# The two single tiles of a fused attention and two-MLP kernel become narrower and join the pairs of the second MLP

## What is computed

```python
qn = q / (norm(q, axis=1) + 1e-6); kn = k / (norm(k, axis=1) + 1e-6)
a = softmax(kn.T @ qn / tau); x = (v @ a)           # [6016, 256]
g = x @ w_gate; x = (silu(g) * (x @ w_val)) @ w_out  # first MLP, 1536 wide
h = x @ w_in2;  out = (h * clip(h + 3, 0, 6) / 6) @ w_out2  # second MLP, 2048 wide
```

## Time and profile before

| | |
|---|---|
| profiled execution | 1092.75 us |
| its span (first to last instruction) | 1090.8 us |
| median of the three timed runs | 1092.9 us |
| PE busy | 1083.8 us (99%), 4890 matmuls |
| DVE, ACT, POOL busy | 787.8, 637.9, 318.3 us |
| DMA | 46.81 MB, of 115417 packets 96528 under 512 B |
| granted TensorE clock | 1.00 |

### The profile page before, as it was taken

The page is one execution under the profiler, slowest core; times in us unless marked ns, Lnnn a source line. Parts: engine busy times, 40 slices in busy tenths (PEclk is TensorE's granted clock), DMA queues, the critical chain, the costliest instruction groups (busy, mean ns, idle before and its releaser), DMA issues.

```text
span 1090.8 us, 14296 instructions
## 1 busy us (share of the span) xinstructions
PE 1083.8 (99%) x4890; PEld 905.2 (83%) x4890; DVE 787.8 (72%) x1160; ACT 637.9 (58%) x1113; POOL 318.3 (29%) x232
## 2 busy tenths in 40 slices
PE   9999999999999999999999999999999999999999
PEld 7888988888888888888877878888888888888888
DVE  6788777667666766756688786776776776776776
ACT  8731245665665566566566776676676676665322
POOL 7999462200210220223087432122121121000000
DMA  9711112002002100101122200020020020020210
GB/s 380 247 34 20 39 34 40 1 1 65 13 1 58 20 1 21 38 1 42 56 59 65 90 1 19 21 39 21 20 39 23 17 39 20 1 40 14 39 20 16
DMA packets 115417, 46.81 MB, mean 43 GB/s; under 512 B 96528, under 2 KB 105104, under 8 KB 115344
## 3 DMA queue, kind: packets, MB, share of 16 engines
q1 hardware_dynamic: 114768, 44.71, 15.2%
q10 hardware_dynamic: 576, 1.18, 0.3%
HBM read 33.55 MB, written 12.32 MB: 42 GB/s over the span
## 4 chain that ended last, share of the span: by engine, by line
PE 95%; DVE 2%; issue 1%; DMA 0%; ACT 0%; ACTq 0%; DVEq 0%
PE psum L1639 42%; PE psum L1650 34%; PE psum L1542 5%; PE psum L1563 4%; PE psum L1552 4%; PE psum L1420 2%; PE psum L1524 2%; PE psum L1596 1%; DVE prod L1146 1%; PE psum L1452 1%; PE psum L1433 0%; PE psum L1594 0%; PE psum L1577 0%; DMA qk_first<-in_k 0%; DVE slots L1274 0%
## 5 line engine op out<-in xcount | busy, mean ns | idle before, releaser
L1650 PE MATMUL psum<-prod,down_w 128*128 128x512 f32 x1680 | 412.9, 389 | 0.0
L1650 PEld LDWEIGHTS psum<-prod,down_w 128*128 128x128 f32 x1680 | 315.4, 188 | 65.5 <-DVE y_right L1298 0.2
L1639 PE MATMUL psum<-x_even,up_w 128*128 128x512 f32 x1092 | 267.0, 390 | 2.7 <-DVE slots L1278 2.6
L1639 PE MATMUL psum<-x_odd,up_w 128*128 128x512 f32 x1008 | 245.5, 390 | 0.5 <-DVE more_slots L1320 0.5
L1639 PEld LDWEIGHTS psum<-x_even,up_w 128*128 128x128 f32 x1092 | 204.2, 188 | 47.3 <-DVE slots L1278 5.0
L1639 PEld LDWEIGHTS psum<-x_odd,up_w 128*128 128x128 f32 x1008 | 189.0, 188 | 40.6 <-DVE more_slots L1320 1.2
L1278 DVE TENSOR_TENSOR slots<-psum,slots 128x512 f32<-128x512 f32 x100 | 68.7, 687 | 55.4 <-ACT slots L921 33.3
L1269 DVE TENSOR_TENSOR slots<-psum,slots 128x512 f32<-128x512 f32 x80 | 55.2, 690 | 73.9 <-PE psum L1639 73.6
L1146 DVE TENSOR_TENSOR prod<-slots,prod 128x512 fp32r<-128x512 f32 x120 | 90.9, 766 | 21.1 <-ACT prod L889 21.1
L1324 DVE SCALAR_TENSOR_TENSOR prod<-slots,prod 128x512 fp32r<-128x512 f32 x120 | 85.8, 715 | 26.5 <-ACT prod L967 22.5
L1320 DVE SCALAR_TENSOR_TENSOR slots<-slots 128x512 f32<-128x512 f32 x100 | 72.2, 722 | 32.0 <-ACT slots L977 32.0
(11 more groups left out here) (177 smaller groups left out, 1403.5 us busy)
## 6 DMA issues: line engine op xcount, KB each, us to landing
out<-out_sb SPq DMA_DIRECT2D x45, 128.0 KB, 2.7
v_in<-in_v SPq DMA_DIRECT2D x44, 128.0 KB, 3.3
qk<-in_q SPq DMA_DIRECT2D x8, 512.0 KB, 9.2
qk<-in_k SPq DMA_DIRECT2D x7, 512.0 KB, 10.7
x_odd_raw<-y_rows SPq DMA_DIRECT2D x12, 256.0 KB, 3.2
y_rows<-act_out SPq DMA_DIRECT2D x10, 256.0 KB, 2.1
y_rows<-y_right SPq DMA_DIRECT2D x10, 256.0 KB, 3.0
x_even_raw<-y_rows SPq DMA_DIRECT2D x10, 256.0 KB, 3.2
```

What stands on the lines that cost most here:

```text
L1639: end = mm(bank, w[:, u, k, part, :], XS[pair % 2][:, k, m, :], start=start and (part, m) == PASSES[0], stop=stop and (part, m) == PASSES[-1],
L1650: end = mm(SUMS_OUT[2 * side + h], w[:, j, part, h * P:(h + 1) * P], buffer_of(f, x)[:, m, :], start=start and (part, m) == PASSES[0], sto ...
```

## The change

The tiles at the two ends of the order become two equal ones: ALONE = (6016 - 10 x 512) / 2 = 448 tokens, at tokens 0 and 448. The ten tiles of the pairs follow them. In the first MLP both still run singly, with 448 where there were 512 and 384. In the second MLP the two form a sixth pair of 448-token tiles, which runs second (pair NARROWER = PAIRS + 1); `second_alone`, `up2`, `down_rows`, `finish_rows` and the weights kept for them (`row2_w`) go away. Every helper of a frame cuts its buffers to `pair_width`. The last pair (LAST_PAIR, 512 tokens wide) now ends the kernel: `finish_second` runs the downs of its last frame, `turn_last` transposes all four sums from PSUM, and `store` writes them, the left tile by SP, the right tile by SP (two DMAs) and ACT (two).

```diff
-    TILES = N // BANK
-    LAST = N - TILES * BANK
+    PAIRS = N // (2 * BANK)
+    ALONE = (N - 2 * PAIRS * BANK) // 2
...
-    FRAMES = SECOND + PAIRS * FRAMES2
+    FRAMES = SECOND + (PAIRS + 1) * FRAMES2
+    NARROWER, LAST_PAIR = PAIRS + 1, 2 * PAIRS
...
+    def pair_width(pair):
+        return ALONE if pair == NARROWER else BANK
...
+        def store(queue, pair, side, groups=range(GROUPS)):
+            queue.wait_ge(out_ready, 2 * KC * (pair - PAIRS) + KC * (side + 1))
+            for g in groups:
+                queue.dma_start(tile(out, tile_of(pair, side))[g],
+                                out_sb[g * SQUARE:(g + 1) * SQUARE, side, 0:pair_width(pair) // SQUARE * KC, :]).then_inc(out_stored, 16)
...
-            load_y_alone(1)
-            store(TILES - 2, 0, 4 * PAIRS - 2)
-            store(TILES - 1, 1, 4 * PAIRS)
-            store(0, 0, 4 * PAIRS + KC)
-            store_block(sp, 1)
+            for pair in range(PAIRS, LAST_PAIR):
+                if pair + 2 <= LAST_PAIR:
+                    load_y(pair + 2 - PAIRS)
+                store(sp, pair, 0)
+                store(sp, pair, 1)
+            store(sp, LAST_PAIR, 0)
+            store(sp, LAST_PAIR, 1, range(2))
...
-            second_alone(0)
-            second_alone(1)
-            act.wait_ge(out_stored, 16 * GROUPS * TILES)
-            for b in range(LAST_BLOCKS):
-                act.wait_ge(low_summed, b + 1)
-                nc.scalar.copy(out_rows(b), ROWS[b][:, C:2 * C]).then_inc(low_kept, 1)
-            for b in (0, 2):
-                store_block(act, b)
+            store(act, LAST_PAIR, 1, range(2, GROUPS))
...
+            def turn_last(side):
+                for h in range(KC):
+                    dve.wait_ge(z_summed, KC * side + h + 1)
+                    nc.vector.transpose(out_sb[:, side, h::KC, :],
+                                        sums_out(LAST_PAIR, side, h).rearrange("p (m t) -> p m t", t=SQUARE)).then_inc(out_ready, 1)
...
-                    mm(bank, w[:, u, k, part, :], XS[pair % 2][:, k, m, :],
+                    mm(bank, w[:, u, k, part, :], XS[pair % 2][:, k, m, 0:pair_width(pair)],
...
+            def finish_second():
+                f = FRAMES - 1
+                for x in ORDER2[:2]:
+                    down_second(f, x)
+                for x in ORDER2[2:]:
+                    side, j = "LR".index(x[1]), J2 - 2 + "12".index(x[0])
+                    pe.wait_ge(high_of[x], FRAMES - SECOND)
+                    pe.wait_ge(low_of[x], FRAMES - SECOND)
+                    for h in range(KC):
+                        for part, m in PASSES:
+                            end = mm(sums_out(LAST_PAIR, side, h), down2_w[:, j, part, h * P:(h + 1) * P], buffer_of(f, x)[:, m, :],
+                                     start=False, stop=(part, m) == PASSES[-1])
+                        end.then_inc(z_summed, 1)
...
-            second_alone(0)
-            second_alone(1)
+            finish_second()
```

More of the change, by code:

```diff
@@ L666, in split_x @@
                     pool.wait_ge(x_high, 7 * pair + k + 1)
-                    high, low = (XS[pair % 2][:, k, part, :] for part in range(2))
+                    high, low = (XS[pair % 2][:, k, part, 0:pair_width(pair)] for part in range(2))
                     nc.gpsimd.tensor_tensor(low, raw_x(pair, k), high.bitcast(fp32), ALU.subtract).then_inc(x_ready, 1)
@@ L749, in _ @@
             split_x(PAIRS + 1)
-            for pair in range(PAIRS + 2, 2 * PAIRS):
+            for pair in range(PAIRS + 2, LAST_PAIR + 1):
                 at = frames_before(pair - 1)
@@ L760, in _ @@
                 split_x(pair)
[L761 to L764, removed]
-                for b in range(KC):
-                    pool.wait_ge(y_alone_high, KC * i + b + 1)
-                    high, low = (XS[i][:, 2 * b, part, 0:alone(i)] for part in range(2))
-                    nc.gpsimd.tensor_tensor(low, y_raw(i, b), high.bitcast(fp32), ALU.subtract).then_inc(y_alone_ready, 1)
         @block.scalar
@@ L920, in first_frame @@
                     act.wait_ge(full["R"], f)
-                nc.scalar.copy(kept7, chain(f)).then_inc(p7_kept, 1)
+                nc.scalar.copy(kept7(f), chain(f)).then_inc(p7_kept, 1)
                 if f == 1:
@@ L943, in cast_down2 @@
                 nc.scalar.copy(down2_w[:, 4 * n:4 * n + 4, 0, :], down2_raw[:, 4 * n:4 * n + 4, 1, :]).then_inc(down2_high, 1)
-            def cast_row2(n):
-                nc.scalar.copy(row2_w[:, 2 * n:2 * n + 2, 0, :], row2_raw[:, 2 * n:2 * n + 2, 1, :]).then_inc(row2_high, 1)
             def keep_z(pair, side):
@@ L956, in keep_z @@
                 for h in range(KC):
-                    nc.scalar.copy(z_kept(pair, side)[:, h, :], SUMS_OUT[2 * side + h]).then_inc(
+                    nc.scalar.copy(z_kept(pair, side)[:, h, :], sums_out(pair, side, h)).then_inc(
                         (z_left_kept, z_right_kept)[side], 1)
@@ L1231, in split @@
[L1231 to L1239 removed]
+                at = c - 4
@@ L1638, in product_of @@
                 for part, m in PASSES:
-                    end = mm(bank, w[:, u, k, part, :], XS[pair % 2][:, k, m, :],
+                    end = mm(bank, w[:, u, k, part, :], XS[pair % 2][:, k, m, 0:pair_width(pair)],
                              start=start and (part, m) == PASSES[0], stop=stop and (part, m) == PASSES[-1],
```

354 lines of the change are left out of this document (97 added, 257 removed).

## The result

The changed kernel takes 1095.71 us (median of 11 runs, 1094.92 to 1096.72) against 1092.91 before (1092.14 to 1093.31): ratio 1.0025, 95% interval 1.0016 to 1.0033, so 1.7 to 3.6 us slower. In a later job, untouched, it took 1095.05 against 1092.62: ratio 1.0023 (1.0014 to 1.0032). The forecast was 1093.1, with a range to 1095.4: no change was expected, and it is slower. The first median lies 0.3 us above the range, the later one inside it.

The account below looks back on a forecast made before the run. PE was taken to bound the kernel, busy 99% of the span. Narrow frames 72.0 plus end 13.8 against 85.3 gave +0.5, with frame 1's -0.3 making +0.2: 1093.1 us, range 1090.6 to 1095.4.

Parts of the forecast that it names:

- 448 is half way: 0.200 us: Matmul cost at 448 tokens, estimated between measured 0.1733 us at 384 and 0.2267 at 512; eight narrow frames take 72.0 us.
- The upper bound of 0.202: Range allowance in case width counts a little in steps: 0.202 us per 448-token matmul, adding 0.7 us.
- First MLP, "nothing in sum", then -0.3: Single tiles' matmuls: -5.8 and +5.8 us cancel; dearer downs cover 0.3 us of frame 1's wait for DVE.
- The sixth pair without a stall: Second MLP's narrow frames cost no stall: 0.3 to 0.4 us left before product 3's or product 2's wait.
- The end: From E, the end of the last frame's products, to the span's end: 13.8 us, including 6.0 us of store data.
- Neither bound: Last stores: lower, ACT's two DMAs cost nothing beside SP's, end at E + 12.2; upper, alternation costs a tenth, +0.6 us.
- The first rival: Last stores hidden or quick, 2.6 us behind the last matmul as now, so the saving stays: 1088.2 us; chance 0.13.
- The second rival: Eight narrow frames each wait for ACT's copy or the clip: +3.3 us, 1096.4; chance 0.11.
- the third: Two queues' last stores disturb each other, 1 MB in 8 us instead of 6: 1095.2 us or more; chance 0.05.

Follow-up runs that it names:

- the widths run: Changed kernel plus 15 groups of 24 matmuls, 256 to 512 tokens wide, behind its last matmul; 448 tokens took 202.9 ns a matmul.
- with 400 tokens: Changed kernel with only the narrow pair's matmuls cut to 400 of 448 tokens, other engines still at 448; 1089.17 us in one execution.
- the run with SP alone: Changed kernel with all four DMAs of the last right tile issued by SP, none by ACT; 1094.58 us.
- the run with long runs: Changed kernel with the last pair stored in 4 KB runs instead of 128 bytes, 1024 output rows in another order; 1092.61 us, ratio 1.0002.
- the mended end: Changed kernel with the last pair's sums copied to SBUF, turned by 16 PE transposes, stored by four DMAs in 1 KB runs; 1094.37 us.

## Why the prediction was wrong

**The step that failed** is "448 is half way: 0.200 us". The mechanism of the sum was right, the term was mis-sized. It was drawn as a line through 256, 384 and 512 tokens; the widths run shows that the line ends at 400. 360 matmuls of the sixth pair at 0.2027 instead of 0.200 are 1.0 us, and that is what the middle row of the first table is over (482.4 for 481.4). The upper bound of 0.202 that I gave to it was too low too. The prediction's own sign of being wrong, narrow frames longer than 9.1 us, came with 9.12. The width ought to have been treated as unseen, with 0.2267 as its end, 9.6 us: too wide a bound to use, but it would have put weight on slower. Of the 2.6 us between forecast and first median this term is 1.0, the part ahead of the second MLP 0.7 and the end 0.4; the rest is mostly that this median lies 0.7 us above the profiled execution, where 0.15 had been taken.

**First MLP, "nothing in sum", then -0.3.** The second MLP starts +0.4 and -0.1 us from its place before in the two profiles, against -0.3. The singles and frames 0 and 1 by themselves, 98.18 us before and 97.99 and 98.00 now, gave -0.2. In the first profile the rest is a first matmul that starts 0.1 us later and 0.5 us in the frames from frame 2 on, whose matmuls are as before. The 432 dearer matmuls, 1.15 us, were not in the sum; the two waits on DVE gave back more than the 0.3 claimed (0.5 at 108.98, 0.65 by the idle entries of frame 1). That part came near by luck: two errors of about 1 us cancel.

**The sixth pair without a stall** held: frames of one length, no idle entry. The spare time was judged rightly: with 400 tokens it is used up in some frames.

**The end** was right within 0.4 us: E + 14.2 for 13.8. PE's wait for 2R, the transposes, the store's first issue (E + 5.83 for 5.65) and the 6.0 us of data at 175 GB/s all came as worked out. The 0.4 us are 0.2 in front of the first store and the rest in the last completion. Neither bound came: the 6.0 us taken between them held, and the second queue adds nothing. That agrees with the Trainium skill, "DMA: Bandwidth & Descriptors", "Issuing engines are not separate DMA queues"; this trace shows it with 6.0 us for 1 MB by two queues, and the run with SP alone with 5.9 by one.

So the answer to where the gain went: before, 82.7 us of matmuls behind the frames of 1005.53; now 73.0 + 6.4. PE is 3.3 us better, and not 4.4. Behind the last matmul 7.8 us pass, where it was 2.6: 5.2 us worse. Together that is 1.9 us; what is left of the two spans' difference lies ahead of the second MLP. The first rival (the saving stays) falls with this; the run with long runs shows what that end costs, 2.4 us of the median, and comes back to the kernel before the change but no lower. The second rival (stalls) and the third (stores disturbing each other) did not occur, though the time came out on their side.

**What stays open.** The spans of the two profiles are 2.4 and 1.8 us above that of before, the medians 2.8 and 2.4. The runs of the changed kernel scatter over 1.8 and 1.4 us, those of before over 1.2. All eleven first runs of the changed kernel lie 1.8 us above their spans, and the spans go from 1093.1 to 1094.9, so this scatter is inside the span. One place of it is shown, the start of the second MLP (596.0 to 597.3); another, the fetch of instructions at the end, is seen with the mended end alone. Which of them moves the medians by another half microsecond was not tried. The 0.3 us by which the first median went past my range are smaller than what is open here, and the later median lies inside it; that it came out slower than forecast holds for both.

No version here that computes the whole result beats the kernel before the change. What was not tried: computing the last frame's left tile by itself, so that its store starts under the right tile's matmuls.

## What to carry to other kernels

A saving on a busy engine must be set against what the change bares at the end: here a whole pair's output, 1 MB in 128-byte runs, costs 6 us that nothing covers, and a frame's chain of copies on top of it. Price a tile width by a run of that width, not by a line between its neighbours: 448 tokens cost 0.453 ns a token, 512 cost 0.443 and 400 cost 0.450. And cheaper matmuls also cover less, while dearer ones beside a wait may be free.

## What the runs showed that I had not expected

- Matmuls with their own weights cost their width plus 32 cycles up to 400 tokens, and 36 to 43 from 416 to 504; in the kernel, 512 is at 32 again.
- With a packet that fetches instructions (16 KB, 1.2 us) amid the last stores, their data trailed off at 25 GB/s for 1.6 us, and the last one landed 1.5 us later than without it.
- 4 KB runs from 32 partitions flowed at some 235 GB/s, 1 KB runs from 128 partitions at about 380, and 1 KB runs from 112 partitions at some 310 with a slow tail.
- In the second MLP, each low part of DVE that began while a POOL operation ran took 1.3 to 1.7 us instead of 0.6, five in the changed kernel's profile and six in that with 400 tokens. It ended 0.01 to 0.4 us behind the POOL operation. Low parts during which a POOL operation began were not slow.
